# Identity transposes into an unread bank between the first layer and the experts of an attention and two-layer kernel

## The chip, the core and the metric

The kernel runs on one core of a Trainium2 chip. Its time is the device time of one execution in microseconds (us), and the median over several executions is compared. TensorE's clock has two levels, 1.2 and 2.4 GHz; the profile gives the granted clock as a share of full speed, so 0.50 is 1.2 GHz and 1.00 is 2.4 GHz.

## What is computed

Sparse attention (a window of 128 keys and 4 sink keys), a first layer with a leaky activation, and then a layer of 8 experts of which each token uses one, with room for 384 tokens in each expert.

```
attn = softmax(mask(q @ k.T / sqrt(D))) @ v            # 2 x 8 heads x 768 x 64
x = rows of attn                                       # 1536 x 512
h = x @ w_in                                           # 512 -> 2048
x = (max(h, 0) + alpha * min(h, 0)) @ w_out            # 2048 -> 512
logits = x @ w_gate                                    # 512 -> 8
expert_idx = argmax(logits, axis=1)
gate_w = softmax(logits) at expert_idx
# the first `capacity` tokens of each expert, in order:
out[i] = gate_w[i] * (relu(x[i] @ w1[e]) @ w2[e])      # 512 -> 1024 -> 512
```

## The kernel before

All tokens are in 12 tiles of 128. Attention and the first layer run interleaved: `each_step` issues, step by step, a piece of attention for a pair of heads, a block of 128 of the 2048 hidden columns (`hidden`) and its share of the first layer's output (`y_sum`). Each float32 operand is split into a high part and the rest, and a product is three fast matmuls (`three`, L802 to L807); ScalarE makes the high parts (L618 for weights, L738 for an expert's tokens) and VectorE the low parts (L1076, L1286).

A finished tile t is then routed in four TensorE steps, `ROUTE` (L955): `y_T` transposes the tile (4 transposes, L800), `logits` multiplies it with `w_gate` (L936, 8 columns wide), `ranks` counts the tokens of each expert ahead (L945, L946, 8 columns), `slots` builds a table from slot to token (L952, 72 columns). Between them VectorE runs `choose` (L1145), `rank` (L1165) and `tables` (L1203), and ScalarE evacuates the transposed tile (L681). Most tiles do this inside the first layer's steps. The last two, tiles 10 and 11, do it after `each_step`, in the two nested loops of L997 to L999: each step for both tiles before the next step. Tile 11 has its own banks and scratch, so that it need not wait for tile 10.

After that comes the passage to the experts. TensorE sums the counts (L1001) and waits for VectorE to copy them to SBUF (L1270, `counts_in_sbuf`). `Busy` (L580) then reads the eight counts into registers of TensorE's own sequencer, one after another (`value_load`, L587), as ScalarE and VectorE do in theirs; later, an expert's second or third tile is skipped if its count is too small. Meanwhile VectorE computes the token numbers (until L1282) and GpSimd gathers the tokens of each tile of an expert by indirect DMA (L549). `slot_T(i)` (L1005) waits for gather i, and for i above 0 also for `x_low2(i - 1)`, since all go through one bank (`O_BANK`), and transposes it with four transposes. `expert_in(0)` (L1013) follows `slot_T(1)`: 24 matmuls with 512 columns, the first of them the first consumer of the split tokens. `hidden_T` and `expert_out` finish an expert's tile. An engine works through its instructions in the order written, and TensorE's sequencer does the register reads in that same order.

`H_BANK[0]` is bank 0: the first layer's even hidden blocks and later the first half of `expert_in(0)` stand there. Nothing reads it in between.

Of the kernel before, what the change touches and what calls it, by code (L numbers as in the profile page):

```python
# [11 lines left out]
P = 128  # L12
# [3 lines left out]
def sparse_attention_then_two_expert_layers(  # L16
# [32 lines left out]
    D = H * DH  # L49
    F1 = w_in.shape[1]  # L50
    E, _, F2 = w1.shape
    N = B * S
    KC = D // P
    NF = F1 // P
# [18 lines left out]
    NC = N // CW  # L73
# [9 lines left out]
    with ctx:  # L83
        def sb(name, shape, dt=F32):
            return ctx.enter_context(nc.sbuf_tensor(name, shape, dt))

        def sem(name):
            return ctx.enter_context(nc.semaphore(name))
# [70 lines left out]
        ident = sb("ident", [P, P])  # L159
# [74 lines left out]
        activation_done = sem("activation_done")  # L234
# [49 lines left out]
        H_BANK, Y_BANK, S_BANK, O_BANK, P_BANK = bk[0:2], bk[2:4], bk[4:6], bk[6], bk[7]  # L284
# [78 lines left out]
        def each_step(step):  # L363

            for i in range(-AHEAD, 0):
                step(-2, NF + i, i + AHEAD)
            for c in range(-1, NC):
                for i in range(NF):
                    step(c, i, H * TPC * (c + 1) + i + AHEAD)
# [13 lines left out]
        def _(sp):  # L383
            def load_piece(p):
                src, _, _, dst, loaded, _ = piece(p)
                first, ring = (NP1, STG2) if p >= NP1 else (0, STG0 if p < FULL0 + STG else STG)
                if p >= first + ring:

                    sp.wait_ge(weights_high_split, p - ring + 1)
                    sp.wait_ge(weights_low_split, p - ring + 1)  # L390
                sp.dma_start(dst, src).then_inc(loaded, 16)
# [221 lines left out]
        def _(act):  # L613
            def weights_high(p):
                _, hf, col, staged, loaded, value = piece(p)
                act.wait_ge(loaded, value)
                wait_half_free(act, p)
                act.copy(wh[:, hf, col:col + PIECE], staged).then_inc(weights_high_split, 1)  # L618
# [179 lines left out]
        def _(pe):  # L798
            def tr(dst, src):
                return pe.transpose(dst, src, ident[:, :])  # L800

            def three(dst, a, b, start, stop):  # L802

                (ah, al), (bh, bl) = a, b
                pe.matmul(dst, ah, bh, start=start, stop=False, skip_group_check=True)  # L805
                pe.matmul(dst, ah, bl, start=False, stop=False, skip_group_check=True)  # L806
                return pe.matmul(dst, al, bh, start=False, stop=stop, skip_group_check=True)  # L807
# [78 lines left out]
            def hidden(m, half):  # L886
                c, f = divmod(m, NF)
                if half == 0:
                    if f == 0:
                        pe.wait_ge(x_low_split, TPC * (c + 1))  # L890
                    if m == 0:
                        pe.wait_ge(alpha_copied, 1)
                    if c == 0 and f % (NF // FP1) == 0:
                        pe.wait_ge(weights_low_split, place_in(KC * (f // (NF // FP1) + 1) - 1) + 1)
                    if m >= 2:
                        pe.wait_ge(activation_done, m - 1)
                x = xT[c % 2]
                for kk in range(half * KC // 2, (half + 1) * KC // 2):
                    col = kk * F1 + f * P
                    r = three(hidden_of(m), (wh[:, 0, col:col + P], wl[:, 0, col:col + P]),  # L900
                              (x[0][:, kk, :], x[1][:, kk, :]), kk == 0, kk == KC - 1)
                if half == 1:
                    r.then_inc(hidden_done, 1)

            def y_sum(m, tt):
                c, f = divmod(m, NF)
                if tt == 0:
                    pe.wait_ge(activation_low_split, m + 1)
                    if c == 0:
                        pe.wait_ge(weights_low_split, place_out(f) + 1)  # L910
                    if f == 0 and c:
                        pe.wait_ge(y_evacuated, TPC * c)
                cs = slice(tt * P, (tt + 1) * P)
                r = three(Y_BANK[tt][:, :], (g_hl[m % 2][:, 0, cs], g_hl[m % 2][:, 1, cs]),
                          (wh[:, 1, f * D:(f + 1) * D], wl[:, 1, f * D:(f + 1) * D]),
                          f == 0, f == NF - 1)
                if tt == TPC - 1:
                    r.then_inc(y_done, 1)
# [75 lines left out]
                    y_sum(m, 1)  # L994

            each_step(step)
            for r in ROUTE:  # L997
                for t in range(NT - TPC, NT):
                    r(t, NH)  # L999

            pe.matmul(P_BANK[:, 0:E], ones[:, :], ohsum[:, :], start=True, stop=True).then_inc(experts_counted, 1)  # L1001
            pe.wait_ge(counts_in_sbuf, 1)
            busy = Busy(pe)

            def slot_T(i):  # L1005
                pe.wait_ge(tokens_gathered[i % GR], 16 * (i // GR + 1))
                if i:
                    pe.wait_ge(slot_x_low_split, i)
                for kk in range(KC):
                    r = tr(O_BANK[:, kk * P:(kk + 1) * P], x_slot[:, i % GR, kk * P:(kk + 1) * P])  # L1010
                r.then_inc(slot_x_transposed, 1)

            def expert_in(i):  # L1013
                e, j = ITEMS[i]
                pe.wait_ge(slot_x_low_split, i + 1)
                if i >= 2:
                    pe.wait_ge(expert_relu_done, i - 1)
                for c in range(2):
                    for kk in range(KC):
                        if j == 0:  # L1020
                            pe.wait_ge(weights_low_split, NP1 + e * PPH + FP2 * kk + c + 1)
                        col = kk * F2 + c * 512
                        cs = slice(kk * P, (kk + 1) * P)
                        r = three(bk[2 * (i % 2) + c][:, :], (eT[i % 2][:, 0, cs], eT[i % 2][:, 1, cs]),
                                  (wh[:, e % 2, col:col + 512], wl[:, e % 2, col:col + 512]),
                                  kk == 0, kk == KC - 1)
                r.then_inc(expert_hidden_done, 1)
# [9 lines left out]
            def expert_out(i):  # L1037
# [11 lines left out]
                              f == 0, f == NF2 - 1)  # L1049
                r.then_inc(expert_out_done, 1)  # L1050

            slot_T(0)
            busy.run(slot_T, 1, slot_x_transposed)
            expert_in(0)
            busy.run(slot_T, 2, slot_x_transposed)
# [295 lines left out]
```

## Time and profile before

| | us |
|---|---|
| median of 3 executions | 673.5 |
| lowest, highest | 670.8, 673.88 |
| profiled execution, its own time | 675.09 |
| its span, first to last instruction | 673.4 |
| TensorE busy in the span | 601.2 (89%) |
| VectorE, ScalarE, GpSimd busy | 372.2, 287.3, 159.0 |
| mean granted clock | 0.966 |

All engines' rows come from that one profiled execution. "Busy" counts the time in which an engine has an instruction under way; for TensorE it says nothing about how many columns these instructions stream, nor at which clock. A row of the order of time has the start, the duration of the group (several instructions of one kind are merged, with x and their number), the engine, the line, what is written and read, and in brackets how long the engine had been idle and who released it. L800 is the line of every transpose. In such a group the instructions overlap by a part of their duration, so the price of one more is the difference between two groups of different length.

### The profile page before, as it was taken

The page shows a single profiled execution, that of the slowest core. Times are in us where ns is not written, and L with a number is a line of the kernel's source. Part 1 is how long each engine was busy: PE and PEld are TensorE (multiplying, and loading weights), DVE is VectorE, ACT ScalarE, POOL GpSimd, SP SyncE. Part 2 cuts the span into 40 slices and gives each one's busy share as a digit, 9 for nine tenths or more (in the row PEclk, how much of TensorE's full clock was granted, in tenths as well). Part 3 has the DMA queues.
Part 4 walks back from the last instruction along what each step waited for, and adds up shares of the span by engine and source line. Part 5 has one row for each costly group of instructions (what it writes and reads, how often), then busy time and mean ns, then how long its engine had stood idle before and what let it go on. Part 6 is the DMA issues. An engine that isn't in the chain of part 4 may idle for free.

```text
span 673.4 us, 11546 instructions
## 1 busy us (share of the span) xinstructions
PE 601.2 (89%) x3759; PEld 503.2 (75%) x3759; DVE 372.2 (55%) x1133; ACT 287.3 (43%) x681; POOL 159.0 (24%) x213
## 2 busy tenths in 40 slices
PE   4678989999999999999999999929999789859993
PEld 3457878888888888888888899728877667647772
DVE  4545777667567656665664455372853644664410
ACT  4644555433344334333432211233864655664520
POOL 5543222222232222222221000031121322330112
PEclk9999999999999999999999999958999898989997
DMA  7520533201020102010000400294875666865100
GB/s 205 142 80 17 157 82 93 64 17 33 18 63 17 32 17 64 17 33 17 33 17 1 157 1 1 68 290 158 273 244 171 212 214 192 288 212 191 63 32 18
DMA packets 73394, 67.36 MB, mean 100 GB/s; under 512 B 43013, under 2 KB 49173, under 8 KB 73329
## 3 DMA queue, kind: packets, MB, share of 16 engines
q1 hardware_dynamic: 69488, 57.76, 27.7%
q0 software_dynamic: 3840, 8.77, 4.5%
q8 instruction: 36, 0.59, 0.4%
q14 instruction: 30, 0.24, 0.1%
HBM read 57.75 MB, written 12.58 MB: 104 GB/s over the span
## 4 chain that ended last, share of the span: by engine, by line
PE 82%; DVE 5%; ACT 4%; issue 4%; DMA 1%; POOL 1%; ACTq 0%; DVEq 0%; POOLq 0%
PE bank L805 21%; PE bank L807 20%; PE bank L806 20%; PE bank L800 9%; PE bank L842 4%; PE bank L868 4%; PE bank L936 2%; ACT fw L639 1%; DMA fw<-y_scratch,v_or_route 1%; DVE rw L1299 1%; ACT wh L618 1%; DVE wl L1076 1%; PE bank L882 1%; DMA o_sb<-in_q_dram 0%; ACT rw L760 0%
## 5 line engine op out<-in xcount | busy, mean ns | idle before, releaser
L805 PE MATMUL bank<-wh,rw 128*128 128x512 f32 x416 | 170.9, 411 | 10.6 <-issue 3.5
L806 PE MATMUL bank<-wl,rw 128*128 128x512 f32 x416 | 165.2, 397 | 0.0
L807 PE MATMUL bank<-wh,rw 128*128 128x512 f32 x416 | 165.1, 397 | 0.0
L1076 DVE TENSOR_TENSOR wl<-fw,wh 128x512 fp32r<-128x512 f32 x160 | 100.2, 685 | 38.0 <-ACT wh L618 36.7
L805 PE MATMUL bank<-rw,wh 128*128 128x256 f32 x384 | 113.2, 295 | 0.0
L807 PE MATMUL bank<-rw,wl 128*128 128x256 f32 x384 | 109.0, 284 | 0.0
L806 PE MATMUL bank<-rw,wh 128*128 128x256 f32 x384 | 108.7, 283 | 0.0
L720 ACT CAST rw<-fw 128x256 fp32r<-128x256 f32 x96 | 39.0, 406 | 151.1 <-DVE fw L1253 151.0
L805 PEld LDWEIGHTS bank<-wh,rw 128*128 128x128 f32 x416 | 80.1, 193 | 28.3 <-issue 10.2
L807 PEld LDWEIGHTS bank<-wh,rw 128*128 128x128 f32 x416 | 79.5, 191 | 17.9
L618 ACT CAST wh<-fw 128x512 fp32r<-128x512 f32 x160 | 88.0, 619 | 6.0 <-DMA fw<-in_moe_w_dram 2.7
L532 POOL TENSOR_SCALAR fw<-fw,rinv 128x256 f32<-128x256 f32 x96 | 89.7, 946 | 0.0
L806 PEld LDWEIGHTS bank<-wl,rw 128*128 128x128 f32 x416 | 79.9, 192 | 12.8
L1248 DVE TENSOR_SCALAR fw<-bank,alpha_sb 128x256 f32<-128x256 f32 x96 | 46.2, 481 | 77.1 <-PE bank L807 77.0
L800 PE MATMUL bank<-ident,fw 128*128 128x128 f32 (+1 forms) x356 | 63.2, 305 | 23.7 <-DMA fw<-y_scratch,v_or_route 9.1
L805 PEld LDWEIGHTS bank<-rw,wh 128*128 128x128 f32 x384 | 73.1, 190 | 2.7
L806 PEld LDWEIGHTS bank<-rw,wh 128*128 128x128 f32 x384 | 73.0, 190 | 1.6
L527 POOL TENSOR_TENSOR fw<-fw,rinv 128x24 f32<-128x24 f32 x48 | 14.1, 294 | 250.1 <-DVE rinv L1122 250.1
L807 PEld LDWEIGHTS bank<-rw,wl 128*128 128x128 f32 x384 | 72.9, 190 | 0.0
L800 PEld LDWEIGHTS bank<-ident,fw 128*128 128x128 f32 (+1 forms) x356 | 42.8, 152 | 36.6 <-issue 14.2
L1259 DVE TENSOR_TENSOR rw<-fw,rw 128x256 fp32r<-128x256 f32 x96 | 43.7, 455 | 35.3 <-ACT rw L720 35.3
L648 ACT COPY fw<-bank 128x512 f32<-128x512 f32 (+1 forms) x48 | 26.5, 551 | 80.5 <-PE bank L800 80.4
(138 smaller groups left out, 654.1 us busy)
## 6 DMA issues: line engine op xcount, KB each, us to landing
fw<-in_moe_w_dram SPq DMA_DIRECT2D x128, 256.0 KB, 4.8
fw<-in_moe_w_in_dram SPq DMA_DIRECT2D x16, 256.0 KB, 3.1
fw<-in_moe_w_out_dram SPq DMA_DIRECT2D x16, 256.0 KB, 2.8
o_sb<-in_q_dram SPq DMA_DIRECT2D x12, 256.0 KB, 3.2
o_sb<-in_k_dram SPq DMA_DIRECT2D x12, 256.0 KB, 3.9
y_scratch<-fw SPq DMA_DIRECT2D x12, 256.0 KB, 2.1
out_dram<-v_or_route SPq DMA_DIRECT2D x12, 256.0 KB, 2.9
v_raw<-in_v_dram SPq DMA_DIRECT2D x11, 256.0 KB, 3.3
```

What stands on the lines that cost most here:

```text
L532: pool.tensor_scalar(x, x, rinv[:, 2 * r + a:2 * r + a + 1], None, ALU.mult).then_inc(prob_normalised, 1)
L618: act.copy(wh[:, hf, col:col + PIECE], staged).then_inc(weights_high_split, 1)
L720: act.copy(g_hl[m % 2][:, 0, :], g_full[:, m % 2, :]).then_inc(activation_high_split, 1)
L800: return pe.transpose(dst, src, ident[:, :])
L805: pe.matmul(dst, ah, bh, start=start, stop=False, skip_group_check=True)
L806: pe.matmul(dst, ah, bl, start=False, stop=False, skip_group_check=True)
L807: return pe.matmul(dst, al, bh, start=False, stop=stop, skip_group_check=True)
L842: m = pe.matmul(S_BANK[a][:, 0:KW], x[ds, :], y[ds, :], start=i == 0, stop=i == 2)
L868: m = pe.matmul(O_BANK[a * DH:(a + 1) * DH, r * P:(r + 1) * P], v_s[:, 2 * r + a, :], pT[:, (2 * s + a) * P:(2 * s + a + 1) * P], start=(r ...
L1076: dve.tensor_tensor(wl[:, hf, col:col + PIECE], staged, f32(wh[:, hf, col:col + PIECE]), ALU.subtract).then_inc(weights_low_split, 1)
L1248: dve.tensor_scalar(g_neg[:, :], hb, 0.0, alpha_sb[:, m % NF:m % NF + 1], ALU.min, ALU.mult).then_inc(negative_part_done, 1)
L1259: dve.tensor_tensor(g_hl[m % 2][:, 1, :], g_full[:, m % 2, :], f32(g_hl[m % 2][:, 0, :]), ALU.subtract).then_inc(activation_low_split, 1)
```

## The change

A helper `keep_busy(k)` issues k transposes of the identity into the first 128 columns of bank 0. It is called before each of the eight routing steps of tiles 10 and 11 (5 before a `y_T`, none before `logits`, 4 before `ranks`, 10 before `slots`), 12 times after the sum of the counts, 46 after the register reads and ahead of `slot_T(0)`, and 14 between `slot_T(0)` and `slot_T(1)`: 110 transposes. A wait for the last read of bank 0 by VectorE stands ahead of the first.

```diff
+            def keep_busy(k):
+
+                for _ in range(k):
+                    tr(H_BANK[0][:, 0:P], ident[:, :])
+
...
             each_step(step)
+            pe.wait_ge(activation_done, NF * NC)
+            filling = {y_T: 5, logits: 0, ranks: 4, slots: 10}
             for r in ROUTE:
                 for t in range(NT - TPC, NT):
+                    keep_busy(filling[r])
                     r(t, NH)
 
             pe.matmul(P_BANK[:, 0:E], ones[:, :], ohsum[:, :], start=True, stop=True).then_inc(experts_counted, 1)
+            keep_busy(12)
             pe.wait_ge(counts_in_sbuf, 1)
             busy = Busy(pe)
...
+            keep_busy(46)
             slot_T(0)
+            keep_busy(14)
             busy.run(slot_T, 1, slot_x_transposed)
             expert_in(0)
```

The order of TensorE's instructions changes at these places alone. At the end of the routing of tiles 10 and 11 it was (bank4 is tile 10's, bank5 tile 11's; bank7 takes the counts; a bracket names the semaphores that the instruction waits for):

```order
L952 MATMUL bank4<-v_or_route 128x72 [waits scores_masked,router_steps]
L952 MATMUL bank5<-mask 128x72 [waits scores_masked,last_tile_router_steps]
L1001 MATMUL bank7<-ohsum,ones 128x8
L587 TENSOR_LOAD counts [waits counts_in_sbuf]
L587 ISA x2
```

and it is, on TensorE at the same place:

```order
L800 MATMUL bank0<-ident 128x128 x10
L957 MATMUL bank4<-v_or_route 128x72 [waits scores_masked,router_steps]
L800 MATMUL bank0<-ident 128x128 x10
L957 MATMUL bank5<-mask 128x72 [waits scores_masked,last_tile_router_steps]
L1009 MATMUL bank7<-ohsum,ones 128x8
L800 MATMUL bank0<-ident 128x128 x12
L587 TENSOR_LOAD counts [waits counts_in_sbuf]
L587 ISA x2
```

Ten transposes now stand ahead of each `slots`, and twelve between the sum of the counts and the first register read. On TensorE from the last register read to the first matmul of the experts it was (bank6 takes the transposed tokens, bank0 is the experts' now):

```order
L587 TENSOR_LOAD counts
L587 ISA x2
L800 MATMUL bank6<-ident,fw 128x128 [waits tokens_gathered0]
L800 MATMUL bank6<-ident,fw 128x128 x3
L594 COMPARE_AND_BRANCH
L800 MATMUL bank6<-ident,fw 128x128 [waits slot_x_low_split,tokens_gathered1]
L800 MATMUL bank6<-ident,fw 128x128 x3
L594 UNCONDITIONAL_BRANCH
L596 UNCONDITIONAL_BRANCH
L805 MATMUL bank0<-wh,rw 128x512 [waits weights_low_split,slot_x_low_split]
```

and it is:

```order
L587 TENSOR_LOAD counts
L587 ISA x2
L800 MATMUL bank0<-ident 128x128 x46
L800 MATMUL bank6<-ident,fw 128x128 [waits tokens_gathered0]
L800 MATMUL bank6<-ident,fw 128x128 x3
L800 MATMUL bank0<-ident 128x128 x14
L594 COMPARE_AND_BRANCH
L800 MATMUL bank6<-ident,fw 128x128 [waits slot_x_low_split,tokens_gathered1]
L800 MATMUL bank6<-ident,fw 128x128 x3
```

The 46 stand behind all eight register reads, and the 14 between the first and the second tile's transposes.

## Rows read from the trace of the kernel before

**Rows 1.** The page: TensorE's busy tenths and granted clock in 40 slices.

```profile
PE   4678989999999999999999999929999789859993
PEclk9999999999999999999999999958999898989997
```

**Rows 2.** Stretches: stretch, length, busy (instructions) by engine, PEclk, DMA share, GB/s.

```profile
436.00:445.00 9.00, 5.31 (x24) 4.82 (x23) 7.07 (x52) 4.93 (x12) 0.00 (x0) 0.51 1.15 344
445.00:451.00 6.00, 0.00 (x0) 0.00 (x0) 5.31 (x12) 0.00 (x0) 3.91 (x3) 0.50 0.61 173
```

**Rows 3.** TensorE in order of time, from the last routing to the end of `expert_in(0)`.

```profile
435.06 2.65 PE L936 MATMUL bank<-wg,fw 128*128 128x8 f32 x16 [0.19 <-ACT fw L681]
...
443.38 0.70 PE L952 MATMUL bank<-mask 128*128 128x72 f32 x2 [1.60 <-DVE mask L1198]
...
451.72 1.11 PE L800 MATMUL bank<-ident,fw 128*128 128x128 f32 x4 [7.32 <-DMA fw<-y_scratch,v_or_route]
454.65 1.11 PE L800 MATMUL bank<-ident,fw 128*128 128x128 f32 x4 [1.82 <-DMA fw<-y_scratch,v_or_route]
455.42 0.77 PE L805 MATMUL bank<-wh,rw 128*128 128x512 f32 x1
...
463.15 0.60 PE L800 MATMUL bank<-ident,fw 128*128 128x128 f32 x4
```

**Rows 4.** TensorE in order of time, the same routing steps of an earlier tile.

```profile
401.85 0.95 PE L936 MATMUL bank<-wg,fw 128*128 128x8 f32 x8
...
408.89 0.44 PE L952 MATMUL bank<-v_or_route 128*128 128x72 f32 x2
```

**Rows 5.** TensorE in order of time, groups of transposes among the experts.

```profile
488.58 1.04 PE L800 MATMUL bank<-ident,fw 128*128 128x128 f32 x8
...
527.94 1.47 PE L800 MATMUL bank<-ident,fw 128*128 128x128 f32 x12
...
555.59 1.94 PE L800 MATMUL bank<-ident,fw 128*128 128x128 f32 x8 [2.14 <-DVE rw L1299]
```

**Rows 6.** Line 587: duration ns min/median/max, first and last start in us.

```profile
L587 PEldq TENSOR_LOAD <-counts x8: 293/305/494, 444.8 to 449.6; - x8
...
L587 PEldq SEQ_ASSERT  x8: 18/18/28, 445.6 to 450.1; - x8
```

**Rows 7.** TensorE resuming after three gaps among the experts, in order of time.

```profile
532.33 1.12 PE L800 MATMUL bank<-ident,fw 128*128 128x128 f32 x4 [2.92 <-DVE rw L1286]
...
557.78 0.76 PE L805 MATMUL bank<-wh,rw 128*128 128x512 f32 x1 [0.25 <-issue]
...
600.76 1.09 PE L800 MATMUL bank<-ident,fw 128*128 128x128 f32 x4 [6.12 <-DVE rw L1286]
```

**Rows 8.** Half-microsecond stretches: the last low one before 460, three with a rise.

```profile
459.50:460.00 0.50, 0.50 (x3) 0.40 (x2) 0.02 (x1) 0.00 (x0) 0.00 (x0) 0.50 0.78 193
...
535.00:535.50 0.50, 0.50 (x4) 0.41 (x3) 0.50 (x2) 0.50 (x2) 0.25 (x1) 0.91 0.01 0
...
559.00:559.50 0.50, 0.50 (x3) 0.42 (x3) 0.50 (x2) 0.50 (x2) 0.39 (x1) 1.00 0.06 17
...
606.50:607.00 0.50, 0.50 (x3) 0.37 (x2) 0.50 (x2) 0.13 (x1) 0.00 (x0) 0.72 0.92 307
```

**Rows 9.** TensorE in order of time: first matmul of an `expert_in`, and what followed it.

```profile
502.84 0.47 PE L805 MATMUL bank<-wh,rw 128*128 128x512 f32 x1 [0.38 <-issue]
...
508.37 1.04 PE L800 MATMUL bank<-ident,fw 128*128 128x128 f32 x8
```

**Rows 10.** VectorE in order of time: start of `choose(11)`, and `x_low2(0)`.

```profile
437.75 0.17 DVE L1154 COPY mask<-bank 128x8 f32<-128x8 f32 x1 [0.43 <-PE bank L936]
...
453.49 0.69 DVE L1286 TENSOR_TENSOR rw<-bank,rw 128x512 fp32r<-128x512 f32 x1 [3.11 <-ACT rw L738]
```

**Rows 11.** The chain that ended last, after `expert_in(1)`: start, us, what.

```profile
469.76 0.40 ACT v_raw L752
...
478.88 0.70 DVE wl L1076
```

## The prediction

> **What bounds the kernel now.** I read the page first: TensorE is busy nine tenths of nearly every slice, and its one empty place in the middle is slice 27 of 40 (437.7 to 454.5 us), the same slice in which the granted clock reads 5 tenths [rows 1]. So TensorE bounds the kernel nearly everywhere, and in this place something else does: the chain of the last two tiles' routing, the token numbers and the gathers. The stretches say more: the clock is at 1.2 GHz (0.51, 0.50) from 436 on, first while TensorE works on narrow matmuls, then while it does nothing for six microseconds [rows 2]. The order of time then shows what this costs: the first `expert_in` begins at 455.42 and ends at 463.15, 7.73 us for 24 matmuls [rows 3], where the same 24 at 2.4 GHz take 508.37 - 502.84 = 5.53 us [rows 9]. The clock was low to 460.0 [rows 8]. That is the cost which a filling of the gap can take away, and it is small: 2.2 us there and a little in the narrow steps.
>
> **What a filling transpose costs.** At 2.4 GHz 12 take 1.47 us and 8 take 1.04, so one more costs 0.108 us; at 1.2 GHz 8 take 1.94 and 4 take 1.12, so one more costs 0.205 [rows 5, 7]. In `slot_T` four take some 0.43 or 0.82 us of path, by the same prices. The 110 are 11.9 us of TensorE's time at the high clock and 22.6 at the low one. All the rest is how much of this lies in waits.
>
> **Part 1, the routing of tiles 10 and 11.** I take for a start that the transposes hold the clock here, since the fall at 436 came after a stretch with few wide instructions, into which ten now go. The 5 before each `y_T` take 0.54 us; the first five lie in the wait for the evacuation, the second five put off `y_T(11)` by about 0.5 us and `logits` by 0.1. `logits` for both tiles is 2.65 us from 435.06, most of it at the low clock [rows 3]; at the high one it is twice 0.79 to 0.95 [rows 4]. It gains little on the path: VectorE's `choose(11)` starts at 437.75, after 0.43 us without work behind `choose(10)` [rows 10]: these 0.43 us go. `ranks` and its fours hide behind `choose` and `rank`. The tens take 1.08 us each and fit: VectorE needs 2.3 us for each `rank`. `slots(11)` goes from 0.70 to 0.44 us [rows 3, 4], 0.26 on the path, and some 0.1 is given back to the second five. Together the counts come some 0.6 us earlier, at 444.1 instead of 444.7.
>
> **Part 2, the twelve.** They stand ahead of the register reads. The sequencer can hand them to the array and start reading, then they cost nothing; or the reads begin only when they are done. The sum of the counts is done near 443.8, the twelve take 1.3 us, to 445.1, and the counts are ready at 444.1: up to 0.9 us later. No row shows which; I take nothing, because the sequencer reads its first count at 444.8, right when the counts come [rows 6], and keep 0.9 for the range.
>
> **Part 3, the register reads.** The idle time of 7.32 us ahead of `slot_T(0)` [rows 3] is not one wait. The eight reads run on TensorE's sequencer from 444.8 to 450.1, 5.3 us [rows 6]. They stay; nothing fills them, since they are themselves what the sequencer does. Only 450.1 to 451.72 is a wait for the gather. With the counts 0.6 us earlier the reads end at 449.5.
>
> **Part 4, the 46.** They begin there. At the high clock they take 46 x 0.108 = 5.0 us, to 454.5. But TensorE has then been idle for some 4.5 us. In the gaps among the experts of 2.92, 2.14 and 6.12 us the clock had fallen by the time work resumed: the transposes behind them, 4 in 1.12 and 1.09 and 8 in 1.94, have the low clock's durations [rows 5, 7]. From the resumption the low clock lasted 535.05 - 532.33 = 2.7 us, 559.0 - 555.59 = 3.4 and 606.8 - 600.76 = 6.0 us [rows 5, 7, 8], and 460.0 - 454.65 = 5.4 in the place itself [rows 3, 8]. I take the middle of these, 4.4 us: 21 transposes at the low clock, 25 at the high (2.7 us), 7.1 us in all, to 456.6. With 2.7 us it is 13 and 33, 6.3 us; with 6.0 us 29 and 17, 7.8 us. So `slot_T(0)` starts at 456.6 (455.8 to 457.3) and not at 451.72, though its tokens are there.
>
> **Part 5, the fourteen and `slot_T(1)`.** Before, `slot_T(1)` came 2.93 us after `slot_T(0)`; it waited for its gather, while `x_low2(0)` was ready at 454.2, 2.5 us after `slot_T(0)` began [rows 3, 10]. At the high clock that is 2.1 us, and the fourteen (1.5 us) with `slot_T(0)`'s own 0.43 lie inside. `slot_T(1)` starts at 458.6 to 458.7 instead of 454.65: **4.0 us late**.
>
> **Part 6, what comes back.** From `slot_T(1)` to the end of `expert_in(0)` it was 463.15 - 454.65 = 8.5 us; at the high clock 0.43 + 5.53 = 5.96, so **2.5 us are gained**. The net is **+1.5 us**; with the ends of part 4 +0.7 to +2.2, and +3.1 with the 0.9 of part 2. The shift then stays: what waits next is the chain through `relu(1)`, the weight splits and `expert_in(3)`, from 469.76 to 479.58 [rows 11], and all of it starts from `expert_in(1)`, so it moves as a whole. Weight transfers do so too, each behind the split that empties its place. The weights of `expert_in(0)` are ready long before: its first matmul follows `slot_T(1)` without a wait [rows 3].
>
> Later gaps are touched by accident only: the three low stretches of [rows 7, 8] cost 2.7 / 2, 3.4 / 2 and 6.0 / 2, about 6 us together, and where the fall and the rise come moves from run to run. This is about the scatter of the times before, 670.8 to 675.09.
>
> **A rule against the change.** The row first: the shortest run of matmuls ahead of a rise is 559.0 - 557.78 = 1.2 us, and it is the one with eight transposes ahead of it; after 600.76, with four, the matmuls ran from 601.5 to 606.8 before the clock rose [rows 5, 7, 8]. That speaks for transposes that count as activity. The Trainium skill, "TensorE: Matmul & The Clock Gate", "Part 4: PE-mode transpose", says otherwise, that the full clock "doesn't engage" for transpose mode. By the row the sum is +1.5 us, by that rule it is that of rival A.
>
> **The rivals.** *A, transposes don't move the clock* (slower). Then the clock falls at 436 as before and stays low. After `logits` ends at 437.7 come 4 (0.8), `ranks(10)` 0.85, 4 (0.8), `ranks(11)` 0.85, 10 (2.05), `slots(10)` 0.4 and 10 (2.05): `slots(11)` starts at 445.5, not 443.38, 2.1 us late. The reads end at 452.2, the 46 take 9.4 us, to 461.6; 0.82 and the fourteen (2.9) bring `slot_T(1)` to 465.3. The 8.5 us behind it stay, so it is +10.7 us: 684.2. It decides as soon as filling lasts longer than the waits, which at the low clock it does three times. The short run at 557.78 speaks against it; chance 0.08.
>
> *B, the clock survives the reads* (a little faster). The rows show the clock low at the end of a gap, not where in it it fell, and a fall needs some idle time; the reads' 4.5 us may be too few in some executions. Then the 46 end at 454.5, `slot_T(1)` starts at 456.6, and the net is 1.95 - 2.5 = -0.6 us: 672.9. The two gaps of 2.92 and 2.14 us, shorter and yet with a low clock behind them, speak against [rows 5, 7]; chance 0.14.
>
> *C, the filling lies in the wait altogether* (faster), if the reads overlap with array work or are much shorter in this order. Then `slot_T(1)` goes by its gather, 0.6 us earlier at 454.05, and the net is -0.6 - 2.5 = -3.1 us: 670.4. The written order speaks against it, since the 46 stand behind the reads; chance 0.08.
>
> *D, the change does nothing that can be seen*: the late `slot_T(1)` and the faster matmuls cancel to within 0.5 us. This is the lower edge of the forecast; chance 0.1.
>
> **The numbers.** The forecast case has the remaining 0.6. Against the profiled execution's own 675.09 it gives 676.6; the scatter between executions is above such a difference, so I put it on the median, 673.5 + 1.5 = 675.0 us. The range reaches from C with a part of the scatter to the upper end of the forecast with the same, 671 to 679; A is left out above. A measurement of this kernel can tell about 0.5%, 3.4 us, from no change. Faster by more than that: C and a lucky B, 0.07. Slower by more: A, and the forecast's upper end with the 0.9 us, 0.15. Within: 0.78.
>
> **What would show it.** Right: the clock at 1.00 from 436 to about 445, at 0.50 somewhere in 447 to 456, the counts 0.6 us earlier, the 46 in 6 to 8 us with the durations changing inside, `slot_T(0)` with no wait ahead of it, and `expert_in(0)` in 5.5 us. Wrong: a wait left ahead of `slot_T(0)` (C), the 46 in 5.0 us (B), the clock low from 436 to beyond 465 (A), or reads of other length than 5.3 us.

## The result, and the profile after

The changed kernel takes **677.68 us** (median of 22 executions, 673.91 to 679.32), the kernel before 674.25 in the same comparison (22 executions, 670.8 to 678.91). The ratio is **1.0048, 95% interval 1.0032 to 1.0064**: 3.2 us slower, between 2.2 and 4.3. The forecast was 675.0, 1.5 us slower, in a range of 671 to 679. The sign and the range held, and the loss was twice the forecast. The medians alone are 3.4 us apart.

The page of the changed kernel has lost its empty slice: where [rows 1] had a 2 in TensorE's row it has a 6, and the clock's 5 has become a 7, since the clock is now low for one stretch of 7 us and not of 24.

```profile
span 676.6 us, 11766 instructions
PE 611.4 (90%) x3869; PEld 513.9 (76%) x3869; DVE 372.4 (55%) x1133; ACT 287.5 (42%) x681; POOL 158.6 (23%) x213
PE   4688989999999999999999999969999789859993
PEclk9999989999999999999999999979999998889998
```

TensorE is busy for 10.2 us more, and the kernel is slower. The stretches of the changed kernel, to set beside [rows 2] (stretch, length, busy and instructions by engine, PEclk, DMA share, GB/s):

```profile
436.00:445.00 9.00, 7.92 (x68) 7.15 (x67) 6.58 (x49) 5.78 (x14) 0.00 (x0) 1.00 1.10 337
445.00:451.00 6.00, 1.20 (x12) 0.96 (x10) 5.71 (x15) 0.00 (x0) 3.48 (x3) 0.83 0.85 229
```

So the routing of the last two tiles now runs at full clock (1.00, was 0.51). In the next six microseconds TensorE still does almost nothing: 1.2 us, the rest of the twelve. That is the register reads. TensorE in order of time, the rows that answer to [rows 3]:

```profile
433.90 0.40 PE L812 MATMUL bank<-wh,rw 128*128 128x512 f32 x1
...
436.45 1.90 PE L941 MATMUL bank<-wg,fw 128*128 128x8 f32 x16
...
444.13 0.44 PE L957 MATMUL bank<-mask 128*128 128x72 f32 x2 [0.77 <-DVE mask L1209]
444.41 0.33 PE L1009 MATMUL bank<-ohsum,ones 128*128 128x8 f32 x2
444.60 1.51 PE L800 MATMUL bank<-ident 128*128 128x128 f32 x12
450.92 7.60 PE L800 MATMUL bank<-ident 128*128 128x128 f32 x46 [4.80 <-issue]
458.35 0.60 PE L800 MATMUL bank<-ident,fw 128*128 128x128 f32 x4
458.79 1.69 PE L800 MATMUL bank<-ident 128*128 128x128 f32 x14
460.44 0.63 PE L800 MATMUL bank<-ident,fw 128*128 128x128 f32 x4
...
466.38 0.60 PE L800 MATMUL bank<-ident,fw 128*128 128x128 f32 x4
```

The 46 begin after 4.80 us of idle time, take 7.6 us, and `slot_T(0)` (458.35) follows without a wait: its gather is long there (in no46 below, with the same routing, it is there 18.7 us behind the first layer's last matmul; here `slot_T(0)` starts at 24.5). The reads themselves, beside [rows 6]:

```profile
L587 PEldq TENSOR_LOAD <-counts x8: 297/305/722, 445.2 to 450.3; - x8
...
L587 PEldq SEQ_ASSERT  x8: 18/18/32, 446.3 to 450.8; - x8
```

**One clock for all traces.** The two profiled executions cannot be compared by their start: the changed one reached the end of the first layer, in code that the change does not touch, 1.25 us later (433.90 against 432.65), and unchanged code differs by as much between three traces of the kernel before (432.15 to 433.88). So every place below is counted from the start of the last matmul of the first layer. *Place* is where `expert_in(0)` is over (the next transposes start), *rest* what the span has behind it. Before: 463.15 - 432.65 = 30.50 and 210.25 us. After: 466.38 - 433.90 = 32.48 and 210.2. The loss of these two traces lies in the place, 2.0 us; the rest is the same.

### The profile page after: what moved, and what is told of

Same layout as the page of the kernel before. It is cut to its first block, busy times and chain, and to the rows that moved or that the text cites. A ratio compares the mean times of both kernels' runs of the same rounds, so it can differ in the third digit from the quotient of the medians.

```text
span 676.6 us, 11766 instructions
## 1 busy us (share of the span) xinstructions
PE 611.4 (90%) x3869; PEld 513.9 (76%) x3869; DVE 372.4 (55%) x1133; ACT 287.5 (42%) x681; POOL 158.6 (23%) x213
## 4 chain that ended last, share of the span: by engine, by line
PE 81%; issue 6%; DVE 6%; ACT 4%; POOL 1%; DMA 0%; ACTq 0%; DVEq 0%; POOLq 0%
PE bank L810 21%; PE bank L812 20%; PE bank L811 19%; PE bank L800 11%; PE bank L847 4%; PE bank L873 4%; PE bank L941 1%; ACT fw L639 1%; DVE wl L1087 1%; ACT wh L618 1%; PE bank L887 1%; DVE fw L1259 0%; DVE rw L1105 0%; DMA o_sb<-in_q_dram 0%; DVE fw L1264 0%
## 5 line engine op out<-in xcount | busy, mean ns | idle before, releaser
L810 PE MATMUL bank<-wh,rw 128*128 128x512 f32 x416 | 170.7, 410 | 10.7 <-issue 6.1
L800 PE MATMUL bank<-ident,fw 128*128 128x128 f32 (+1 forms) x356 | 61.3, 298 | 14.2 <-issue 7.2
L800 PEld LDWEIGHTS bank<-ident,fw 128*128 128x128 f32 (+1 forms) x356 | 41.5, 148 | 26.5 <-issue 14.8
L648 ACT COPY fw<-bank 128x512 f32<-128x512 f32 (+1 forms) x48 | 26.5, 552 | 80.7 <-PE bank L800 80.6
```

## The experiments

Each kernel was compared with the kernel before on the same chip.

| kernel | ratio to before, 95% interval | place us | rest us |
|---|---|---|---|
| before, three traces | | 30.50, 29.28, 29.49 | 210.3, 209.9, 210.0 |
| changed, two traces | 1.0048 (1.0032 to 1.0064) | 32.48, 32.57 | 210.2, 210.3 |
| no46 | 0.9994 (0.9965 to 1.0023) | 28.26 | 211.0 |
| only46 | 1.0041 (1.0022 to 1.0061) | 32.59 | 208.0 |
| fill24 | 0.9997 (0.9978 to 1.0017) | 30.00 | 206.7 |
| fill92, twice | 1.0169 (1.0138 to 1.0201), 1.0147 (1.0111 to 1.0183) | 37.08, 37.52 | 211.5, 211.8 |
| spread5, twice | 0.9974 (0.9954 to 0.9993), 0.9986 (0.9959 to 1.0012) | 27.39, 27.14 | 211.7, 211.4 |
| spread_trim | 0.9983 (0.9960 to 1.0005) | 27.32 | 211.4 |
| spread_only | 0.9992 (0.9965 to 1.0019) | 28.76 | 209.7 |

### Which part loses: no46 and only46

My theory T: the 46 stand behind the register reads, run past the gather, and lose more than they give back. The rival R: the loss comes from the other 64 transposes.

```diff
-            keep_busy(46)
             slot_T(0)
```

> The changed kernel without the 46 transposes ahead of slot_T(0); all other filling stays. Theory T (the 46 stand behind the register reads and run past the gather, the rest of the filling costs nothing): slot_T(0) starts again with its gather, some 7.2 us after the counts; the clock is at 1.00 until about 445, falls in the idle reads and rises only in expert_in(0). Time -0.5 to +0.5 us against the kernel before, 3 us below the changed kernel. Rival R (the loss comes from the routing's filling, the twelve or the fourteen, and the 46 are paid back by the faster expert_in(0)): no gain over the changed kernel, some 3 us slower than the kernel before.

Measured 673.96 us, ratio 0.9994 (0.9965 to 1.0023), as T said, and the place is 28.26, 4.2 us before the changed kernel's. TensorE in order of time in that kernel:

```profile
444.96 1.51 PE L800 MATMUL bank<-ident 128*128 128x128 f32 x12
452.99 1.12 PE L800 MATMUL bank<-ident,fw 128*128 128x128 f32 x4 [6.52 <-DMA fw<-y_scratch,v_or_route]
453.90 2.87 PE L800 MATMUL bank<-ident 128*128 128x128 f32 x14
456.60 0.60 PE L800 MATMUL bank<-ident,fw 128*128 128x128 f32 x4
```

`slot_T(0)` waits for its gather again. The fourteen run at low clock (2.87 us for 14, where the changed kernel has 1.69) and put `slot_T(1)` off (22.3 us behind the last first-layer matmul, where the kernel before has 21.5 to 22.0), but the clock is up again at 456.3, ahead of `expert_in(0)`. The place is 1.5 us before the mean of the kernel before and the whole time is the same: this trace has a rest of 211.0 us.

The other half, the 46 alone (against the changed kernel):

```diff
-            filling = {y_T: 5, logits: 0, ranks: 4, slots: 10}
+            filling = {y_T: 0, logits: 0, ranks: 0, slots: 0}
...
-            keep_busy(12)
...
-            keep_busy(14)
```

> The kernel before with the 46 transposes ahead of slot_T(0) alone. Theory T: the clock is low from 436, the 46 start at 450.1 and take 7 to 8 us, slot_T(0) starts near 457.5 and slot_T(1) 2.1 us later, 5 us late, of which the warm expert_in(0) gives 2.5 back: 2.5 to 3.5 us slower than the kernel before, as slow as the changed kernel. Rival R: as fast as the kernel before or up to 1 us faster.

Measured 676.47 us, ratio 1.0041 (1.0022 to 1.0061), 1.5 to 4.1 us slower, and the place 32.59 is the changed kernel's. T holds and R falls: the 46 alone are as slow as all 110.

### How the loss grows with the number: fill24 and fill92

```diff
-            keep_busy(46)
+            keep_busy(24)
```

> The changed kernel with 24 in place of 46 transposes ahead of slot_T(0). Theory T: all 24 run at the low clock, 0.205 us each, 4.9 us from 17.0 us behind the last first-layer matmul, so slot_T(0) starts at 22.0 and expert_in(0) ends at 30.0 us behind it, where the three traces of the kernel before have 29.8 on average: 0 to +1 us against the kernel before. Rival (the loss is in what follows and not in the number of transposes): as slow as the changed kernel, 3 us.

Measured 674.99 us, ratio 0.9997. In the trace the 24 start 17.0 us behind the last first-layer matmul, take 5.12 us and end in `slot_T(0)` at 455.72 - 433.77 = 21.95; the place is 30.00, as expected to the tenth:

```profile
450.77 5.12 PE L800 MATMUL bank<-ident 128*128 128x128 f32 x24 [4.80 <-issue]
455.72 0.60 PE L800 MATMUL bank<-ident,fw 128*128 128x128 f32 x4
```

Doubled instead:

```diff
-            keep_busy(46)
+            keep_busy(92)
```

> The changed kernel with 92 in place of 46 transposes ahead of slot_T(0). The added ones come after the clock has risen, at 0.108 us each. Theory T (all on the path): 46 x 0.108 = 5.0 us slower than the changed kernel, 8.2 slower than the kernel before. Rival R (the 46 still lie partly in a wait): less than 4 us slower than the changed kernel.

Measured 685.05 us on 4 executions, ratio 1.0169: 11.4 us slower (9.3 to 13.5) than before, where T said 8.2. The 92 take 12.20 us against 7.60 for 46, so 46 more cost 4.6 us there, all on the path, and the place is 37.08. The rival, under 4 us above the changed kernel, falls. The sign and the place are T's; the whole time is not. So the same kernel ran again.

> The kernel of fill92 once more, with more executions, since the first four lay 11.4 us above the kernel before (9.3 to 13.5) where its trace showed expert_in(0) only 7.3 us late. Theory T: the time above the kernel before comes down to what the place shows and the scatter of the later falls allows, 7 to 9.5 us. Rival (a longer delay costs something more, later): 10 us or more again, and a second trace shows over 1 us more from the end of expert_in(0) to the end of the span than the kernel before has, 210.0 us.

Measured 684.61 us on 6 executions, ratio 1.0147 (7.5 to 12.3 us slower): the medians are 10.7 us apart, the ratio gives 9.9, and the second trace has a rest of 211.8 us. By what I had written this is the rival, if barely. The place explains 37.3 - 29.8 = 7.5 us, the rest 1.6 more. In both its traces the clock falls four times among the experts (near 539, 563, 587 and 608), where every trace of the kernel before has three falls. What a fourth one costs is taken up below; why it comes remains without an explanation. Another 1 to 2 us are in no trace: both traced executions are the fastest of their four and six (683.06 and 682.98 us against medians of 685.05 and 684.61).

### Is it the same in every execution: three more traces

My sum had read the low clock's end from one execution.

> The kernel before, unchanged, for a second trace. Theory P (my sum read the low clock's end in expert_in(0), 460.0, from one execution, and where the clock falls and rises moves against the program from execution to execution): the clock rises somewhere between 457 and 460 us, counted as in the first trace, and expert_in(0) takes 6.2 to 7.7 us, on average about 6.9, so that the warm expert_in(0) gives back 0.8 us less than I took. Rival Q (it is the same in every execution): the rise is at 460.0 and expert_in(0) takes 7.7 us again.

> The kernel before, unchanged, for a third trace. Theory P: a third place of the rise between 457 and 460 us and another length of expert_in(0) between 6.2 and 7.7 us. Rival Q: 460.0 and 7.7 us again.

> The changed kernel, unchanged, for a second trace. Theory P: the 46 take between 6.3 and 8.2 us, with the rise at another place inside them, and expert_in(0) 5.5 us. Rival Q: 7.6 us again, with the rise 4.8 us after their start. Both: the clock rises while nothing but transposes run.

In these traces of the kernel before the clock rose at 459.3 and 457.7 us, which is 25.4 and 25.6 behind the last first-layer matmul; in the first trace it was 27.3. The rise of the second trace, between a low stretch and a full one:

```profile
451.00:459.00 8.00, 4.74 (x15) 3.79 (x16) 2.66 (x6) 3.08 (x6) 3.94 (x4) 0.50 0.92 325
459.00:459.50 0.50, 0.50 (x4) 0.36 (x3) 0.50 (x2) 0.16 (x1) 0.00 (x0) 0.74 0.65 205
459.50:460.50 1.00, 1.00 (x6) 0.83 (x5) 0.72 (x2) 0.00 (x0) 0.00 (x0) 1.00 0.86 205
```

From `slot_T(1)` to the place it took 7.78 and 7.74 us there, and 8.50 in the trace that I had. Theory P holds for the kernel before: I had the longest of three. For the changed kernel P is not borne out: its second trace has 7.67 us for the 46, the rise 5.0 us behind their start and the place at 32.57 against 32.48, which fits the rival as well.

### Do transposes raise the clock

This needed no run of its own. In the changed kernel nothing but transposes runs from 450.92 to 460.8, and the clock rises in the middle of the 46:

```profile
450.50:455.50 5.00, 4.58 (x22) 4.59 (x23) 0.31 (x1) 0.00 (x0) 2.18 (x2) 0.50 0.96 344
455.50:456.00 0.50, 0.50 (x5) 0.50 (x4) 0.00 (x0) 0.00 (x0) 0.00 (x0) 0.71 1.06 422
456.00:458.00 2.00, 2.00 (x21) 2.00 (x19) 0.00 (x0) 0.00 (x0) 0.00 (x0) 1.00 0.72 287
```

22 instructions in 4.6 us, then 21 in 2.0: the price of one falls from 0.21 to 0.10 us. In only46 the clock rose at 454.0, 5.0 us into its own 46. Rival A is refuted. The Trainium skill, "TensorE: Matmul & The Clock Gate", "Part 4: PE-mode transpose", says that the full clock does not engage for transpose mode; these float32 transposes of an identity show the opposite: 0.50 to 1.00 while nothing else ran.

### A filling that costs nothing: spread5 and its variants

If TensorE's array can work through transposes while its sequencer reads registers, the filling belongs between the reads. The transposes then lie in 5.3 us that are lost anyway.

```diff
-            def __init__(self, eng):
+            def __init__(self, eng, between=lambda: None):
...
-                self.count = [eng.value_load(counts[0:1, e:e + 1], min_val=0, max_val=N) for e in range(E)]
+                self.count = []
+                for e in range(E):
+                    self.count.append(eng.value_load(counts[0:1, e:e + 1], min_val=0, max_val=N))
+                    between()
...
-            busy = Busy(pe)
+            busy = Busy(pe, lambda: keep_busy(5))
...
-            keep_busy(46)
+            keep_busy(8)
```

> The changed kernel with the 46 taken apart: 5 transposes behind each of the eight register reads of TensorE's sequencer, and 8 more ahead of slot_T(0). Theory T (the sequencer hands them to the array and goes on reading, so that the array works during the reads): reads still end near 450, slot_T(0) starts with its gather, the clock stays at 1.00 from the first layer on, expert_in(0) takes 5.5 us; 2.5 to 3.5 us faster than the kernel before. Rival S (a register read waits until the array is done with what stands ahead of it): the reads take 0.5 us longer each, 4 us in all, and the time is 1 to 2 us above that of the kernel before.

Measured 673.70 us, ratio 0.9974 (0.9954 to 0.9993): 0.5 to 3.1 us faster than the kernel before, 1.8 by the ratio, less than T's 2.5 to 3.5. The medians are only 0.1 us apart (673.70 and 673.80); four of its twelve executions lie under 672 us, where the kernel before has three of 29, and the ratio reflects these, so the gain in whole time is not firm. TensorE in order of time, and the reads:

```profile
444.54 1.51 PE L803 MATMUL bank<-ident 128*128 128x128 f32 x12
446.28 6.36 PE L803 MATMUL bank<-ident 128*128 128x128 f32 x48 [0.24 <-issue]
452.74 0.66 PE L803 MATMUL bank<-ident,fw 128*128 128x128 f32 x4
453.23 1.69 PE L803 MATMUL bank<-ident 128*128 128x128 f32 x14
455.25 0.66 PE L803 MATMUL bank<-ident,fw 128*128 128x128 f32 x4 [0.33 <-issue]
```

```profile
L589 PEldq TENSOR_LOAD <-counts x8: 296/305/732, 445.2 to 450.4; - x8
...
L589 PEldq SEQ_ASSERT  x8: 18/26/32, 446.2 to 450.9; - x8
```

The reads end at 450.9 as in the changed kernel (450.8), though 40 transposes stand between them, so a read does not wait for the array. Rival S is refuted. The eight reads last 5.8 us against 5.6 in the changed kernel, so the 40 transposes cost them 0.2 us here. The stretches of this kernel from 436 to 460 all have the clock at 1.00:

```profile
436.00:445.00 9.00, 7.92 (x67) 7.14 (x66) 6.65 (x50) 5.70 (x14) 0.00 (x0) 1.00 1.12 344
445.00:451.00 6.00, 5.76 (x45) 4.49 (x43) 5.64 (x15) 0.00 (x0) 3.54 (x3) 1.00 0.77 227
451.00:460.00 9.00, 8.57 (x55) 7.36 (x55) 3.79 (x6) 3.25 (x6) 3.62 (x4) 1.00 0.88 312
```

The place is 27.39, 3.1 us before the first trace of the kernel before and 2.4 before the mean of its three. That is what rival C of the prediction would have been, by another way. Once more, with a shorter variant beside it:

> The kernel of spread5 once more, on another occasion, beside its shorter variant. Theory T: the clock at 1.00 from the first layer through expert_in(0), which ends 27.4 us behind the last first-layer matmul; 1 to 3 us faster than the kernel before. Rival (its gain was the chance place of the later falls of the clock): no difference from the kernel before.

> spread5 with 4 in place of 12 transposes ahead of the first register read and 3 in place of 8 behind the last. Theory T: the first read is no longer slowed by 0.25 us and slot_T(0) starts with its gather: the clock stays at 1.00 and expert_in(0) ends 0 to 0.5 us sooner than in spread5, 27.0 us behind the last first-layer matmul; 2 to 3 us faster than the kernel before. Rival: the thinner filling lets the clock fall in the reads, and expert_in(0) ends 1 to 2 us later than in spread5.

```diff
-            keep_busy(12)
+            keep_busy(4)
...
-            keep_busy(8)
+            keep_busy(3)
```

(Against spread5.) Measured 673.82 and 673.49 us beside 674.71 of the kernel before, ratios 0.9986 (0.9959 to 1.0012) and 0.9983 (0.9960 to 1.0005), both intervals with 1. The places, 27.14 and 27.32, are again 2.5 us early, as T said; the whole gain is 0.9 to 1.2, and the rival of spread5_again, no difference in the whole time, is not excluded. The trim made no difference to the place, and T was wrong about its first read: behind four transposes it takes 692 ns, where spread5 had 732 and 644 behind twelve.

> The kernel before with 5 transposes behind each register read, 8 ahead of slot_T(0) and 14 ahead of slot_T(1), and no filling in the routing or ahead of the reads. Theory T: the clock falls at 436 as before, the reads' filling, at the low clock 1.03 us per five against 0.66 us per read, piles up to some 2 us until the clock has risen, so that slot_T(0) starts 0 to 1.5 us behind its gather; expert_in(0) is warm: -1.0 to -2.5 us against the kernel before. Rival (the routing's filling is what pays in the version with both): no faster than the kernel before.

```diff
-            filling = {y_T: 5, logits: 0, ranks: 4, slots: 10}
+            filling = {y_T: 0, logits: 0, ranks: 0, slots: 0}
...
-            keep_busy(12)
```

(Against spread5.) Measured 673.95 us, ratio 0.9992 (0.9965 to 1.0019). The clock is low from 438.5 to 452; the 48 take 8.18 us and `slot_T(0)` starts 20.7 us behind the last first-layer matmul, where spread5 has 18.9. The place is 28.76, 1.0 us early instead of 2.4. So the routing's filling is worth 1.4 us of place once the reads are filled too. The whole time, 0.5 us faster by the ratio where T said 1.0 to 2.5, can't tell this from nothing.

**Where the gain of spread5 goes.** In its three traces the rest is 211.4 to 211.7 us, 1.4 to 1.7 longer than in the kernel before. The same gap ahead of an `expert_in`, 2.65 us idle in every one of them, shows one part of it. The kernel before, first trace, then its second trace, then spread5, in order of time:

```profile
580.40 0.50 PE L805 MATMUL bank<-wh,rw 128*128 128x512 f32 x1 [2.65 <-DVE rw L1286]
580.73 0.40 PE L806 MATMUL bank<-wl,rw 128*128 128x512 f32 x1
```

```profile
579.06 0.80 PE L805 MATMUL bank<-wh,rw 128*128 128x512 f32 x1 [2.65 <-issue]
579.65 0.63 PE L806 MATMUL bank<-wl,rw 128*128 128x512 f32 x1
```

```profile
578.57 0.73 PE L813 MATMUL bank<-wh,rw 128*128 128x512 f32 x1 [2.65 <-issue]
579.10 0.63 PE L814 MATMUL bank<-wl,rw 128*128 128x512 f32 x1
```

0.40 us for a matmul is the high clock's duration, 0.63 the low one's: the clock outlived the gap in the first and fell at its end in the other two; in spread5 it came back only at 582.1. A stretch of 3.4 us at low clock costs 1.7, about what the rest is longer by.

The second and third trace of the kernel before have this fall too, at 578.7 and 577.2, but they miss the one near 532, which its first trace has. So all three have three falls among the experts, and the changed kernel has three in both traces, while the two traces of spread5, the one of its trim, the one of no46 and the two of fill92 have four. Wherever there are several traces of one kernel the number is the same in all of them, and it is not shown that the fourth fall is chance; that the filling has ended 120 us earlier does not exclude that the earlier place brings it. On the other side, two of spread_trim's twelve executions took 670.7 and 670.8 us at a mean clock of 0.985 and 0.984, and six took 673.9 to 675.0 at 0.980 and 0.981, so executions of one kernel do differ in how long the clock was low. Over all traces the rest runs from 206.7 us (fill24, with two falls among the experts) to 211.8. What decides each fall was not tested, and so it stays open whether a later fall gives the gain back in general or did so in these three traces.

## Why the prediction was right, and what was mis-sized

In places behind the last first-layer matmul (432.65 in the trace that I worked from):

| step | forecast | changed kernel, two traces | kernel before, three traces |
|---|---|---|---|
| last read over (parts 1 to 3) | 16.9 | 17.0, 17.0 | 17.5, 17.0, 17.0 |
| low clock inside the 46 (part 4) | 4.4 us | 4.9, 5.0 us | |
| `slot_T(0)` | 23.9 | 24.5, 24.5 | 19.1, 18.9, 18.5 |
| `slot_T(1)` (part 5) | 26.0 | 26.5, 26.6 | 22.0, 21.5, 21.8 |
| from there to the place (part 6) | 5.96 us | 5.94, 5.94 us | 8.50, 7.78, 7.74 us |
| place | 31.9 to 32.0 | 32.5, 32.6 | 30.5, 29.3, 29.5 |

- **Parts 1 to 3** held as a sum. The clock stayed at 1.00 through the routing, and VectorE's copy of the counts (L1281) starts 11.0 us behind the last first-layer matmul in both traces of the changed kernel, against 11.9, 11.3 and 11.3 in the kernel before: 0.5 us earlier on average, where 0.6 was forecast. The first of the three is the late one because the clock fell at 436.1, inside its `logits` (2.65 us); in the other two it fell behind them (1.95 us). The twelve cost 0.2 us and not 0 or 0.9: the first of the eight reads takes 722 and 751 ns where the three traces of the kernel before have 494, 489 and 493. So the reads last 5.6 us and not 5.3, and they are over at 17.0, which two traces of the kernel before reach as well.
- **Part 3**, that the reads stay and can't be filled, was right for this change and wrong as a general sentence: "nothing fills them, since they are themselves what the sequencer does". The sequencer reads, and the array still works through what it was given. spread5 puts 40 transposes into them for 0.2 us.
- **Part 4** was the right mechanism, half a microsecond short: the low clock lasted 4.9 and 5.0 us behind the reads, not the 4.4 taken from four other resumptions. With fill24 (4.7) and the two traces of fill92 (4.0 and 5.3) beside them, 4.4 lies inside the scatter.
- **The mis-sized terms.** The place in the changed kernel was forecast to 0.6 us, and these 0.6 are the 46, which began 0.2 late and took 0.4 longer. The larger miss is in the kernel before, with which I compared: its place is 29.8 on average and not 30.5. The 8.5 us of part 6 belong to one execution; two more have 7.78 and 7.74, on average it is 8.0, so 2.1 us come back and not 2.5. And `slot_T(1)` stood there at 21.8 on average and not at 22.0, so that it is 4.8 us late and not 4.0. All in all the change costs 32.5 - 29.8 = **2.8 us** at the place, against 1.5 forecast, of which 0.7 is the one trace and 0.6 the 46. 2.8 is inside the measured 2.2 to 4.3.
- **The whole time** in its range of 671 to 679 says little by itself: the range is 8 us wide for a change of 3.2 us, and the 673.5 on which the forecast stands, a median of three, lay 0.75 us under the median of 22. What the forecast earned is the sign and the steps of the table.
- **Downstream** the shift stayed, as said: the rest is 210.2 and 210.3 us against 209.9 to 210.3. In only46, with the same place, it is 208.0, and the third low stretch among the experts lasts 3.4 us there and not 6.8; so an unchanged rest is in part luck.
- **Rival A** fell by the rise inside the 46. **Rival B** did not occur in two traces: the clock fell during the reads both times (at 449.0 and 447.3), and so it did in the traces of no46, fill24 and fill92, which leave the reads unfilled as well. **Rival C** needed another kernel.

## What to carry to other kernels

- Before filling a wait of TensorE, find out what the wait is made of: a gap "until the gather" was for three quarters a row of register reads on TensorE's own sequencer, and what is written behind them starts after them. Fill in the order of the sequencer, between the reads, not behind.
- Filling at the low clock costs twice as much as at the high one (0.21 and 0.10 us for a transpose here), and in all six traces with a filled routing and unfilled reads TensorE resumed at the low one, after 4.6 to 6.5 us of idle time. Count the filling at that price against what the wait has left.
- A clock's rise and fall read from one trace is one draw. Take two or three traces before a term of a microsecond is built on it.

## What was not expected of the hardware

- Transposes alone brought TensorE's clock from 1.2 to 2.4 GHz, 4.9 and 5.0 us after they began in the changed kernel and 4.0 to 5.3 us in its variants with 24 and 92.
- TensorE's array and its sequencer's register reads overlap: eight reads took 5.6 to 5.8 us with transposes ahead of them and between them, 5.4 to 5.6 with the twelve ahead alone and 5.3 with none. The first read behind a run of transposes is slower, 0.59 to 0.75 us against 0.49.
- The clock can outlive an idle gap of 2.65 us in one execution and fall in the same gap in two others of the same kernel (at 578.7 and 577.2). In the first trace of the kernel before it was still at full speed 5 us into the gap of 6.12 us:

```profile
598.00:599.00 1.00, 0.00 (x0) 0.00 (x0) 0.51 (x2) 1.00 (x3) 0.97 (x1) 1.00 1.08 318
599.00:600.00 1.00, 0.00 (x0) 0.00 (x0) 1.00 (x3) 0.18 (x1) 0.69 (x2) 0.97 0.89 301
600.00:601.00 1.00, 0.24 (x1) 0.27 (x2) 0.61 (x2) 0.00 (x0) 0.70 (x2) 0.50 0.94 328
```
